# A float32 chain of attention and two expert mixtures: the first mixture by Strassen's block product, token groups outside and experts inside

## The chip, the cores and the metric

The kernel runs on one core of one Trainium2 chip. The metric is the device time of one execution in microseconds (us), taken as the median of several runs. The engines are TensorE (PE, whose weight loads the profile lists as PEld), VectorE (DVE), ScalarE (ACT), GpSimd (POOL) and SyncE (SP, which here only issues DMAs).

## The reference

2304 tokens of 512 features pass through three parts. The first is a causal attention without softmax with a decay per head. Its output `x` goes through a dense mixture of 8 experts, whose weights `P` come from 8 rounds of row and column normalisation. The result goes through a mixture in which each token visits only its best expert.

```python
attn_out = _attn_ref(q, k, v)                      # B, H, S, DH = 4, 8, 576, 64
x = attn_out.transpose(0, 2, 1, 3).reshape(B * S, H * DH)       # 2304 x 512

# first mixture, E = 8, F = 1024: every token through every expert
logits = x @ w_gate
P = np.exp(logits - logits.max())
for _ in range(8):
    P /= P.sum(1, keepdims=True) + 1e-09
    P /= P.sum(0, keepdims=True) + 1e-09
    P *= N / E
for e in range(E):
    out += P[:, e:e + 1] * (np.maximum(x @ w1[e], 0.0) @ w2[e])

# second mixture: every token through its best expert alone
expert_idx = np.argmax(logits2, axis=1)
for e in range(E):
    mask = expert_idx == e
    out[mask] = gate_w[mask, None] * (np.maximum(x[mask] @ w1[e], 0.0) @ w2[e])
```

## The kernel before

All matrix products of the first mixture, and the second product of the second mixture, are made from two float32r halves of each operand: a rounded part (names with H) and the rest (names with L). One product of two tiles costs three matmuls, H by H, H by L and L by H. ACT writes the H part with a copy or a relu, and DVE or POOL subtracts it from the source for the L part.

**First mixture.** The 16 units are half experts (512 of the 1024 hidden features), in the order expert outside, half inside. Each unit runs over 6 blocks of 384 tokens (`BLK`, `NB`). For a block, `hidden` (L1005 to L1012) makes 4 hidden tiles of 128 features, each from 12 matmuls of 384 columns, and `output` (L1014 to L1024) makes 3 output tiles of 128 tokens, each from 12 matmuls of 512 columns. That is 48 and 36 matmuls per block, 96 blocks in all. ACT's `relu_hi` (L535 to L539) writes `HH` from PSUM, DVE's `relu_lo` writes `HL` (L729) and then adds the weighted output tile in PSUM to `acc` (L757). The weights of the next unit are loaded by SP as one MB for each of `w1raw` and `w2raw` (L319, L320) and split by ACT (L553, L556) and by POOL's `split_lo` (L419, L421). Weights are loaded and split once.

**Normalisation of P.** It runs beside blocks 0 to 5 of the first unit. DVE makes row sums and column partials, and POOL adds the partials over the 128 partitions with `partition_all_reduce` (L436), eight times. After every second one POOL also splits a quarter of the next unit's weights:

```python
for it in range(SINK):
    pool.wait_ge(s_cp, it + 1)
    nc.gpsimd.partition_all_reduce(cs[:, :], cp[:, :], P, bass.bass_isa.ReduceOp.add).then_inc(s_cs, 1)
    if it % 2 == 1:
        split_lo(1, 1, it // 2)
```

**Routing.** In the last unit, after block i, the 3 token tiles of block i-1 are complete. PE transposes them and makes the logits, DVE chooses the expert (`choose`) and ranks the tokens (`rank`), and POOL scatters the rows to their sorted places in DRAM.

**Second mixture.** Tokens lie sorted by expert in tiles of 128, 22 tiles in this run. A tile costs PE 32 float32 products (recorded as 64 matmuls, L1082), 4 transposes of the next tile, and 24 matmuls of 512 columns (L1093 to L1095). Expert weights (`Wa`, `Wb`) sit in 2 slots. When a slot's `Wb` has arrived, ACT writes `WbH` (L596), and DVE and POOL each write four of the eight `WbL` blocks (L306), right ahead of the expert's tiles. Waits are counted semaphores on each engine, in an order written out by hand. SP's waits and DMAs are one queue in order.

Of the kernel before, what the change touches and what calls it, by code (L numbers as in the profile page):

```python
# [13 lines left out]

B, H, S, DH = 4, 8, 576, 64
P = 128
D = H * DH
# [8 lines left out]
FH = F // 2  # L45
NF = FH // P
NT = N // P
BLK = 384
NB = N // BLK
TPB = BLK // P  # L50
# [3 lines left out]
SQ = 32  # L54
# [5 lines left out]
PICK = NB - 2  # L60
assert P < PICK * BLK // E


def tables():

# [13 lines left out]
    row = np.concatenate([(E - np.arange(E)).astype(float), thr, N * np.arange(E), np.arange(TAB)])  # L79
    keep = np.concatenate([np.eye(P), (p[:, None] < p[None, :]), np.ones((P, P)),  # L80
                           np.tile(row, (P, 1))], 1)
# [3 lines left out]
def build(nc, qk, kv, wg1, w11, w12, wg2, w21, w22, attn_tab, keep_tab, out):  # L85
    ctx = ExitStack()
    with ctx:
# [7 lines left out]
        at_w = base  # L95
        WSLOT = 4 * 4 * NF * D
        at_x = at_w + 2 * WSLOT
        at_acc = at_x + 2 * 4 * ND * N
        at_raw = at_acc + -(-4 * NT * ROW // 32) * 32
        at_h = at_raw + 2 * 4 * NF * D  # L100
        at_small = at_h + 2 * 4 * NF * BLK

        W1H, W1L, W2H, W2L = [], [], [], []
        a = at_w
        for s in range(2):
            for name, group in (("W1H", W1H), ("W1L", W1L), ("W2H", W2H), ("W2L", W2L)):
                t, a = place(f"{name}{s}", [P, ND, FH], F32R, a)
                group.append(t)
        XH, a = place("XH", [P, ND, N], F32R, at_x)
        XL, a = place("XL", [P, ND, N], F32R, a)  # L110
        acc, _ = place("acc", [P, NT, ROW], F32, at_acc)
        w1raw, a = place("w1raw", [P, ND, FH], F32, at_raw)
        w2raw, a = place("w2raw", [P, NF, D], F32, a)
        HH, a = place("HH", [P, NF, BLK], F32R, at_h)
        HL, a = place("HL", [P, NF, BLK], F32R, a)
# [3 lines left out]
        a = at_acc  # L119
# [3 lines left out]
        for c in range(4):  # L123
            t, a = place(f"QK{c}", [P, 2, G, C], F32, a)
            QK.append(t)
        assert a <= at_raw
        a = at_h + 2 * 4 * ND * P
        for c in range(4, NC):
            t, a = place(f"QK{c}", [P, 2, G, C], F32, a)
            QK.append(t)  # L130
        assert a <= at_small
        a = at_w + WSLOT
        VD, QT, ST, PT, qd = [], [], [], [], []
        for s in range(3):
# [3 lines left out]
            QT.append(t)  # L138
        for s in range(2):
# [4 lines left out]
        for c in range(1, NC):  # L144
            t, a = place(f"qd{c}", [P, G, C], F32, a)
            qd.append(t)
# [1027 lines left out]
```

## Time and profile before

| | us |
|---|---|
| median of 3 runs | 2081.91 |
| lowest, highest | 2078.32, 2091.56 |
| the profiled execution's own time | 2079.77 |
| its span, first to last instruction | 2078.1 |
| PE busy | 2035.7 |
| DVE, ACT, POOL busy | 658.1, 357.7, 310.0 |

The span is what the rows are measured in. The profiled execution takes 1.7 us more than its span. PE's busy time counts overlapping matmuls once, so the duration of one matmul is longer than the distance to the next one, and only the distance between starts tells what a row of matmuls costs. The execution has three stages: attention to 104 us, first mixture to 1736 us, second mixture to the end.

### The profile page before, as it was taken

The numbers are of one execution on the slowest core, as the hardware profiler recorded it, in microseconds if no ns is written. First come the engines' busy times: TensorE is split into PE (matmuls) and PEld (weight loads), VectorE is DVE, ScalarE is ACT, GpSimd is POOL, SyncE is SP. The second block draws the span as 40 slices with busy tenths as digits, with TensorE's granted clock in tenths as the row PEclk, the third lists the DMA queues.
The fourth block names the chain that finished last, engine by engine and source line by source line (L and its number), as shares of the span: only waits on it lengthen the run. The fifth ranks groups of instructions, "written<-read, shape, count | busy, mean of one in ns | idle before, by whom it ended". The sixth has DMA issues, their size and how long they took to land. (4 is left out here: it accounts for less than half of the span.)

```text
span 2078.1 us, 31657 instructions
## 1 busy us (share of the span) xinstructions
PE 2035.7 (98%) x11660; PEld 1836.6 (88%) x11661; DVE 658.1 (32%) x1223; ACT 357.7 (17%) x715; POOL 310.0 (15%) x288
## 2 busy tenths in 40 slices
PE   8999999999999999999999999999999998999997
PEld 7899999888889999988889999998888987998886
DVE  4444332222222222222222222222222346223554
ACT  2311111111111111111111111111111112002121
POOL 5501101010101010101000000001010012112232
PEclk9999999999999999999999999999999999999998
DMA  9701040104000410221031104010400006114452
GB/s 251 207 0 41 0 147 0 40 0 147 3 37 29 118 40 0 70 77 40 0 111 36 40 0 147 0 40 0 147 0 0 16 31 224 40 40 160 147 202 92
DMA packets 63308, 141.44 MB, mean 68 GB/s; under 512 B 6254, under 2 KB 6254, under 8 KB 63280
## 3 DMA queue, kind: packets, MB, share of 16 engines
q1 hardware_dynamic: 58240, 125.56, 19.2%
q0 software_dynamic: 5040, 15.51, 2.2%
q8 instruction: 17, 0.28, 0.1%
q14 instruction: 11, 0.09, 0.0%
HBM read 92.91 MB, written 49.19 MB: 68 GB/s over the span
## 5 line engine op out<-in xcount | busy, mean ns | idle before, releaser
L1009 PE MATMUL bank<-XH,W1H 128*128 (+1 forms) x1536 | 515.7, 336 | 0.0
L1010 PE MATMUL bank<-XL,W1H 128*128 (+1 forms) x1536 | 514.3, 335 | 0.0
L1011 PE MATMUL bank<-XH,W1L 128*128 (+1 forms) x1536 | 513.8, 335 | 0.0
L1022 PE MATMUL bank<-W2H,HL 128*128 128x512 f32 x1152 | 459.1, 398 | 0.0
L1021 PE MATMUL bank<-W2L,HH 128*128 128x512 f32 x1152 | 453.9, 394 | 0.0
L1020 PE MATMUL bank<-W2H,HH 128*128 128x512 f32 x1152 | 453.1, 393 | 0.0
L729 DVE SCALAR_TENSOR_TENSOR HL<-bank,HH 128x384 fp32r<-128x384 f32 x384 | 213.7, 557 | 577.8 <-ACT HH L539 535.4
L539 ACT ACTIVATE HH<-bank 128x384 fp32r<-128x384 f32 x360 | 177.2, 492 | 1266.9 <-PE bank L1011 1266.9
L757 DVE SCALAR_TENSOR_TENSOR acc<-bank,Pw,acc 128x512 f32 x252 | 180.3, 751 | 521.1 <-PE bank L1022 519.5
L1009 PEld LDWEIGHTS bank<-XH,W1H 128*128 128x128 f32 x1536 | 288.3, 188 | 4.2
L1010 PEld LDWEIGHTS bank<-XL,W1H 128*128 128x128 f32 x1536 | 288.4, 188 | 4.0
L1011 PEld LDWEIGHTS bank<-XH,W1L 128*128 128x128 f32 x1536 | 288.4, 188 | 0.0
L419 POOL TENSOR_TENSOR W1L<-w1raw,W1H 128x512 fp32r<-128x512 f32 x64 | 82.5, 1288 | 1260.0 <-ACT W2H L556 1232.1
L1021 PEld LDWEIGHTS bank<-W2L,HH 128*128 128x128 f32 x1152 | 216.3, 188 | 51.4
L1022 PEld LDWEIGHTS bank<-W2H,HL 128*128 128x128 f32 x1152 | 216.2, 188 | 50.2
L1020 PEld LDWEIGHTS bank<-W2H,HH 128*128 128x128 f32 x1152 | 216.2, 188 | 48.1 <-issue 1.0
L1082 PEld LDWEIGHTS bank<-x2T,Wa 128*128 128x128 f32 x1408 | 162.1, 193 | 6.2 <-issue 3.7
L1082 PE MATMUL bank<-x2T,Wa 128*128 128x128 f32 x1408 | 162.8, 277 | 4.2 <-DVE x2T L816 4.2
L421 POOL TENSOR_TENSOR W2L<-w2raw,W2H 128x512 fp32r<-128x512 f32 x64 | 82.1, 1283 | 0.0
L1093 PE MATMUL bank<-WbH,hH 128*128 128x512 f32 x176 | 75.7, 430 | 0.1
L1094 PE MATMUL bank<-WbL,hH 128*128 128x512 f32 x176 | 72.9, 414 | 0.0
L1095 PE MATMUL bank<-WbH,hL 128*128 128x512 f32 x176 | 72.5, 412 | 0.0
(149 smaller groups left out, 1007.6 us busy)
## 6 DMA issues: line engine op xcount, KB each, us to landing
sorted_rows<-blank SPq DMA_DIRECT2D x147, 257.0 KB, 8.7
w1raw<-in_moe_w SPq DMA_DIRECT2D x16, 1024.0 KB, 5.1
w2raw<-in_moe_w SPq DMA_DIRECT2D x16, 1024.0 KB, 8.0
Wa<-in_moe_w SPq DMA_DIRECT2D x8, 2048.0 KB, 7.8
Wb<-in_moe_w SPq DMA_DIRECT2D x8, 2048.0 KB, 10.0
QK<-qk SPq DMA_DIRECT2D x24, 384.0 KB, 9.0
KV<-kv SPq DMA_DIRECT2D x24, 384.0 KB, 10.0
nxt<-sorted_rows POOLq DMA_DIRECT2D x23, 257.0 KB
```

The source lines that it names most:

```text
L419: nc.gpsimd.tensor_tensor(W1L[s][:, j, :], w1raw[:, j, :], W1H[s][:, j, :].bitcast(F32), ALU.subtract).then_inc(s_wlo, 1)
L421: nc.gpsimd.tensor_tensor(W2L[s][:, j, :], w2raw[:, j, :], W2H[s][:, j, :].bitcast(F32), ALU.subtract).then_inc(s_wlo, 1)
L539: nc.scalar.activation(HH[:, j, :], bank[j][:, 0:BLK], ACT.Relu).then_inc(s_hhi, 1)
L729: nc.vector.scalar_tensor_tensor(HL[:, j, :], bank[j][:, 0:BLK], 0.0, HH[:, j, :].bitcast(F32), ALU.max, ALU.subtract).then_inc(s_hlo, 1)
L757: nc.vector.scalar_tensor_tensor(tile, bank[L2B[j]][:, :], weight, tile, ALU.mult, ALU.add).then_inc(s_acc, 1)
L1009: mm(bank[j][:, 0:BLK], W1H[s][:, a, f], xh, start=(a == 0), stop=False)
L1010: mm(bank[j][:, 0:BLK], W1H[s][:, a, f], xl, start=False, stop=False)
L1011: last = mm(bank[j][:, 0:BLK], W1L[s][:, a, f], xh, start=False, stop=(a == ND - 1))
L1020: mm(dst, HH[:, j, tok], W2H[s][:, j, :], start=(j == 0), stop=False)
L1021: mm(dst, HH[:, j, tok], W2L[s][:, j, :], start=False, stop=False)
L1022: last = mm(dst, HL[:, j, tok], W2H[s][:, j, :], start=False, stop=(j == NF - 1))
L1082: last = mm(bank[j // 4][:, (j % 4) * P:(j % 4 + 1) * P], Wa[s][:, a, j * P:(j + 1) * P], x2T[:, a, :], start=(a == 0), stop=(a == ND - 1))
```

## The change

The first mixture is rewritten. The tokens are grouped into 3 groups (`SB`) of 768, the group loop is outside and the expert loop inside. A group consists of two halves of `W` = 384 tokens from different batches. A step handles one group, one expert and a quarter of the hidden features (256). There are 3 x 8 x 4 = 96 steps (`K`). In a step the 256 x 768 hidden block is made by Strassen's scheme (in Winograd's form) over 2 x 2 blocks: 7 block products of 2 x 3 matmuls of 384 columns. The sums of tokens are made once per group (DVE's `x_term`, ACT's `x_hi`, DVE's `x_lo`, POOL's `next_x`). The sums of weights are made in each step by POOL (`w1_sum`), since each weight is now loaded and split three times, once per group. DVE adds the products up with 5 additions per step (`sums_before`, `sums_after`), and the second product of a step is issued inside the next step (`outputs(k - 1, ...)`). It adds only 256 features per pass, so `acc` is updated 6 times per step.

```diff
+            def product(b, s, i, start):
+                for c in range(NK):
+                    blk = WBLK[i][c]
+                    mm(bank[b][:, 0:W], W1H[s][:, blk, :], XH[i][:, c, :], start=start and c == 0, stop=False, ...
+                    mm(bank[b][:, 0:W], W1H[s][:, blk, :], XL[i][:, c, :], ...
+                    last = mm(bank[b][:, 0:W], W1L[s][:, blk, :], XH[i][:, c, :], ...
...
+            def step(k, q, sb=None, route=None, sorted_tile=False):
+                pe.wait_ge(s_w1l, 3 * (k + 1))
+                if not first:
+                    pe.wait_ge(s_hlo, 4 * k - 3)
+                product(BA, s, 0, True).then_inc(s_p1, 1)
+                if not first:
+                    pe.wait_ge(s_c21, k)
+                product(BB, s, 1, True).then_inc(s_p6, 1)
+                if not first:
+                    pe.wait_ge(s_c12, k)
+                product(BC, s, 2, True)
+                pe.wait_ge(s_cs1, k + 1)
+                product(BA, s, 3, False).then_inc(s_p2, 1)
+                pe.wait_ge(s_u2, k + 1)
+                product(BB, s, 4, False).then_inc(s_p7, 1)
+                if not first:
+                    pe.wait_ge(s_hlo, 4 * k)
+                    pe.wait_ge(s_w2l, k)
+                    for t in range(TS):
+                        outputs(k - 1, 1 - s, t, not fixed(k, 1))
+                pe.wait_ge(s_c22, k + 1)
+                product(BC, s, 5, False).then_inc(s_p3, 1)
+                product(BB, s, 6, False).then_inc(s_p4, 1)
```

DVE's order in a step, shortened:

```diff
+            def sums_before(k):
+                dve.wait_ge(s_p6, k + 1)
+                nc.vector.tensor_tensor(c12[:, :], cs1[:, :], bank[BB][:, 0:W], ALU.add).then_inc(s_u2, 1)
+                dve.wait_ge(s_p7, k + 1)
+                nc.vector.tensor_tensor(c22[:, :], cs1[:, :], bank[BB][:, 0:W], ALU.add).then_inc(s_v, 1)
+                nc.vector.tensor_tensor(c22[:, :], c22[:, :], bank[BC][:, 0:W], ALU.add).then_inc(s_c22, 1)
+            def sums_after(k):
+                dve.wait_ge(s_p3, k + 1)
+                nc.vector.tensor_tensor(c12[:, :], c12[:, :], bank[BC][:, 0:W], ALU.add).then_inc(s_c12, 1)
+                dve.wait_ge(s_p4, k + 1)
+                nc.vector.tensor_tensor(c21[:, :], cs1[:, :], bank[BB][:, 0:W], ALU.add).then_inc(s_c21, 1)
+            def hidden_lo(k, i):
+                source = (bank[BA][:, 0:W], c22[:, :], c12[:, :], c21[:, :])[i]
+                dve.wait_ge(s_hhi, 4 * k + i + 1)
+                nc.vector.scalar_tensor_tensor(HL[:, i, :], source, 0.0, HH[:, i, :].bitcast(F32), ...
...
+            # step: sums_before(k); gather 0 to 2 of step k-1; hidden_lo(k, 0); gather 3 to 5;
+            #       hidden_lo(k, 1); sums_after(k); hidden_lo(k, 2); hidden_lo(k, 3)
```

POOL's step prepares the weights of step k+1 and the second weights of step k. `column_sum` is the `partition_all_reduce`. In steps 0, 1 and 2 it is called 2, 3 and 3 times:

```diff
+            def step(k, q, sink=()):
+                sink = list(sink)
+                for i in range(4):
+                    w1_sum(k + 1, i)
+                if sink:
+                    column_sum(sink.pop(0))
+                for i in range(2):
+                    w1_lo(k + 1, (q + 1) % 2, i)
+                if sink:
+                    column_sum(sink.pop(0))
+                w2_lo(k, q % 2)
+                if sink:
+                    column_sum(sink.pop(0))
+                w1_lo(k + 1, (q + 1) % 2, 2)
...
+                    step(step_no(sb, 0, q), q, ((0, 1), (2, 3, 4), (5, 6, 7), ())[q] if sb == 0 else ())
```

SP's loads are now one pair of 512 KB per step, in this order, with five or six of the blank rows' DMAs behind each pair for 28 steps of the first group:

```diff
+            def load_pair(sb, e, q):
+                k = step_no(sb, e, q)
+                sp.wait_ge(s_w1l, 3 * k - 1)
+                load_w1(e, q)
+                sp.wait_ge(s_w2l, k)
+                load_w2(e, q)
...
+                    for i in range(q * FILL // NQ, (q + 1) * FILL // NQ):
+                        sp.dma_start(sorted_rows[...], blank[:, :]).then_inc(s_blank, 16)
```

The gate's logits are no longer made from float32r halves with the gate weights stationary. They are plain float32 products with the tokens stationary and 8 columns moving, 8 calls after each of the last six attention chunks and 24 behind them (72 in all, `gate`), and they land token by token, so DVE's transposes fall away. The attention's output is kept in float32 (`Xf`). Routing works per half group (6 of them). Four are done in the steps q = 1, 2 of the second and third group, two after the last step.

In the second mixture the weights have three slots. DVE makes all eight `WbL` blocks of expert p+2 behind the tiles of expert p, and POOL makes them only for the first expert:

```diff
-                    split_w2_lo(pool, r * 2 + s, s, 0)
-                    send_tiles(r * 2 + s)
...
+                if p + 2 < E:
+                    split_w2_lo(p + 2)
```

## Rows read from the trace of the kernel before

**Rows 1.** The page: busy time and its share of the span, by engine.
```profile
PE 2035.7 (98%) x11660; PEld 1836.6 (88%) x11661; DVE 658.1 (32%) x1223; ACT 357.7 (17%) x715; POOL 310.0 (15%) x288
```

**Rows 2.** Windows: stretch, length, busy us (PE, PEld, DVE, ACT, POOL), clock, DMA share, GB/s.
```profile
0.00:104.20 104.20, 94.23 (x1325) 84.77 (x1327) 47.77 (x104) 34.90 (x78) 58.90 (x64) 0.92 0.86 228
104.20:1620.00 1515.80, 1515.80 (x7611) 1368.12 (x7610) 421.03 (x731) 241.48 (x485) 155.59 (x129) 1.00 0.14 45
1736.00:1763.20 27.20, 21.32 (x139) 18.47 (x139) 19.49 (x52) 5.63 (x12) 10.17 (x10) 0.94 0.47 172
1907.30:2078.10 170.80, 144.26 (x919) 128.83 (x917) 86.85 (x101) 37.45 (x68) 53.39 (x49) 0.91 0.47 164
```

**Rows 3.** Timeline of PE, one block: start, duration (us), engine, line, operation.
```profile
154.38 0.34 PE L1009 MATMUL bank<-XH,W1H 128*128 x1
...
162.73 0.40 PE L1020 MATMUL bank<-W2H,HH 128*128 128x512 f32 x1
...
171.13 0.34 PE L1009 MATMUL bank<-XH,W1H 128*128 x1
```

**Rows 4.** Groups by line: busy us, mean ns of one | idle before.
```profile
L729 DVE SCALAR_TENSOR_TENSOR HL<-bank,HH 128x384 fp32r<-128x384 f32 x384 | 213.7, 557 | 577.8 <-ACT HH L539 535.4 <-ACT HH L587 42.4
L757 DVE SCALAR_TENSOR_TENSOR acc<-bank,Pw,acc 128x512 f32 x252 | 180.3, 751 | 521.1 <-PE bank L1022 519.5
L419 POOL TENSOR_TENSOR W1L<-w1raw,W1H 128x512 fp32r<-128x512 f32 x64 | 82.5, 1288 | 1260.0 <-ACT W2H L556 1232.1 <-issue 27.8
L553 ACT ACTIVATE W1H<-w1raw x56 | 34.9, 624 | 0.0
```

**Rows 5.** Timeline of POOL and DVE between two all-reduces, idle before in brackets.
```profile
140.50 1.28 POOL L419 TENSOR_TENSOR W1L<-w1raw,W1H 128x512 fp32r<-128x512 f32 x1 [6.97 <-issue]
140.61 0.43 DVE L720 TENSOR_REDUCE cp<-Pw 128x8 f32<-128x144 f32 x1
...
148.87 0.42 POOL L436 PARTITION_ALL_REDUCE cs<-cp  x1 [5.83 <-issue]
152.05 0.40 POOL L436 PARTITION_ALL_REDUCE cs<-cp  x1 [2.75 <-DVE cp L720]
```

**Rows 6.** POOL's sequencer at L436, and at L419.
```profile
L436 POOLq MODIFY_POOL_CONFIG  x6: 1/4/4, 143.2 to 181.4; - x6
L419 POOLq MODIFY_POOL_CONFIG  x8: 88/88/88, 133.5 to 190.5; - x8
```

**Rows 7.** DVE's and POOL's weight splits side by side at one change of expert.
```profile
L306 DVE TENSOR_TENSOR WbL<-Wb,WbH x32: 676/685/5884, 1737.2 to 2059.1; 128x512 fp32r<-128x512 f32 x32
...
1909.69 5.88 DVE L306 TENSOR_TENSOR WbL<-Wb,WbH 128x512 fp32r<-128x512 f32 x1
...
1910.06 4.95 POOL L306 TENSOR_TENSOR WbL<-Wb,WbH 128x512 fp32r<-128x512 f32 x4
```

**Rows 8.** Timeline of DVE, results of three tiles in a row.
```profile
1894.27 0.74 DVE L833 TENSOR_SCALAR y<-bank,held 128x512 f32<-128x512 f32 x1
...
1907.34 0.74 DVE L833 TENSOR_SCALAR y<-bank,held 128x512 f32<-128x512 f32 x1
...
1924.66 0.74 DVE L833 TENSOR_SCALAR y<-bank,held 128x512 f32<-128x512 f32 x1
```

**Rows 9.** DMA issues: count, KB each, median us from issue to landing.
```profile
sorted_rows<-blank SPq DMA_DIRECT2D x147, 257.0 KB, 8.7
w1raw<-in_moe_w SPq DMA_DIRECT2D x16, 1024.0 KB, 5.1
w2raw<-in_moe_w SPq DMA_DIRECT2D x16, 1024.0 KB, 8.0
```

**Rows 10.** Timeline: a hand-over from PE to ACT, and the logits of one block.
```profile
1718.93 0.60 PE L1049 MATMUL bank<-ktab,acc 128*128 128x128 f32 x4
1719.13 0.49 ACT L587 ACTIVATE HH<-bank 128x384 fp32r<-128x384 f32 x1 [1.49 <-PE bank L1011]
...
1724.13 2.81 PE L1057 MATMUL bank<-x2c,wg2s 128*32 128x128 f32 x24
```

More of the change, by code:

```diff
@@ L59, with fixed @@
 WARM = 14
-PICK = NB - 2
-assert P < PICK * BLK // E
+PICK = NG - 2
+assert P < PICK * W // E
+NP = 7
+WBLK = ((0, 2), (8, 9), (6, 7), (1, 3), (10, 11), (12, 13), (4, 5))
+def fixed(number, value):
+    return isinstance(number, int) and number == value
 def tables():
@@ L109, in build @@
[L109 to L115, printed above, removed]
+        WB = 4 * D * F // P
+        W1SLOT = 2 * 4 * 2 * NP * P
+        at_sums = base + W1SLOT
+        at_raw = at_sums + 4 * 4 * NK * P
@@ new lines, in _ @@
+            for sb in range(SB):
+                for q in range(NQ):
+                    k = step_no(sb, 0, q)
+                    step(k, q, first=(k == 0), route=2 * sb - 3 + q if sb > 0 and q in (1, 2) else None,
+                         late_x=sb if q == 0 else None)
+                with act.Fori(1, E - 1) as e:
+                    for q in range(NQ):
+                        step(step_no(sb, e, q), q)
+                for q in range(NQ):
+                    step(step_no(sb, E - 1, q), q, last=(q == NQ - 1), sb=sb)
@@ L611, in _ @@
[L611 to L624 removed]
+            relu2_hi(0, (0,))
@@ new lines, in _ @@
+            for t in range(NT - TS, NT - TPB):
+                routing_x(t)
+            routing_exp(NG - 2)
+            for t in range(NT - TPB, NT):
+                routing_x(t)
+            routing_exp(NG - 1)
+            relu2_hi(0, (1,))
+            split_w2_hi(1)
+            act.wait_ge(s_bounds, 1)
+            for p in range(E):
+                start = act.value_load(bounds[0:1, p:p + 1], min_val=1, max_val=MAXT)
+                end = act.value_load(bounds[0:1, p + 1:p + 2], min_val=2, max_val=MAXT)
+                with act.Fori(start, end) as i:
+                    relu2_hi(i, (0, 1))
+                if p + 2 < E:
+                    split_w2_hi(p + 2)
@@ L881, in _ @@
+            dve.wait_ge(s_acc, TS * (K - 1))
+            for t in range(TS - 1):
+                gather(SB - 1, K - 1, E - 1, t, "add")
+            relu2_lo(0, (0,))
+            choose(NG - 2)
+            gather(SB - 1, K - 1, E - 1, TS - 1, "add")
+            rank(NG - 2)
+            choose(NG - 1)
+            rank(NG - 1)
             dve.wait_ge(s_count, 1)
-            link(nc.vector.tensor_copy(count[:, :], bank[7][:, 0:E]))
+            link(nc.vector.tensor_copy(count[:, :], bank[RB][:, COUNT0:COUNT0 + E]))
@@ L1041, in _, with gate @@
-            unit(E - 1, 0)
-            def routing_T(t, dst):
-                pe.wait_ge(s_acc, (2 * E - 1) * NT + t + 2)
+                    chunk(b, c, True)
+            def gate(t):
+                half, at = t % TS // TPB, t % TPB * P
+                for a in range(ND):
+                    last = mm(bank[RB][:, t * E:(t + 1) * E], Xf[t // TS][:, a, half, at:at + P], wgraw[:, a, :],
+                              start=(a == 0), stop=(a == ND - 1), skip_group_check=True)
+                return last
```

1085 lines of the change are left out of this document (623 added, 462 removed).

## The prediction, made before the changed kernel ran

> **What bounds the kernel now.** I read the page first: PE is busy 98% of the span, DVE 32%, POOL 15% [rows 1]. The windows by stage come next. The first mixture lasts from 104.2 to 1736 us, and in its long part PE is busy in every microsecond at a clock of 1.00 [rows 2]. The timeline of PE gives the price of a matmul there. A block runs from 154.38 to 162.73 with 48 matmuls of 384 columns and to 171.13 with 36 of 512, so one costs 8.35/48 = 0.174 us and 8.40/36 = 0.233 us [rows 3]. Blocks of 16.75 us times 96 are 1608 us, and routing beside the last unit makes up the rest. Only fewer matmul slots shorten this stage. Two places matter for what the change may lose. POOL's waits on nothing visible stand beside the all-reduces [rows 5, 6], and DVE and POOL get into each other's way at changes of expert [rows 7, 8]. The last stretch, with seven changes of expert, has a clock of 0.91 and gaps on PE [rows 2].
>
> **1. Matmuls saved.** A step makes 7 x 6 = 42 matmuls of 384 columns and 36 of 512: 42 x 0.174 + 36 x 0.233 = 15.71 us in place of 16.75. Over 96 steps that is -100 us. The operands keep their shapes, so I take the same price.
>
> **2. POOL's all-reduces, steps 0 to 2.** In rows 5, DVE's partial sums are ready at 141.04 and POOL's subtraction pair ends at 143.0, yet the all-reduce stands at 148.87, 5.83 us later, behind no wait. The other way, from an all-reduce to a subtraction, 6.97 us pass. An all-reduce directly after another has no such gap: at 152.05 it waited for DVE alone. POOL's sequencer shows a MODIFY_POOL_CONFIG at exactly these changes, 6 and 8 of them [rows 6]. So each change of kind on POOL costs 5.9 or 7.0 us. Before, PE had six blocks (100 us) of work with weights already split. Now each of the eight all-reduces stands between elementwise work on which the next step's first matmul waits (`s_w1l`).
>
> POOL's subtraction of 512 elements takes 1.29 us [rows 4], thus 0.7, 1.3, 2.5 us for 256, 512, 1024. From the first maximum (gmx) to W1 of step 1: 0.4 + 7.0 + sums 2.7 + (5.9 + 0.4) + (7.0 + 1.9) + (5.9 + 0.4) + (7.0 + 2.5) + 2.5 = 43.6 us. Step 1 has three all-reduces: 2.7 + 6.3 + 8.9 + 6.3 + 9.5 + 6.3 + 9.5 = 49.5, and 2.5 for weights that are only requested when `w2_lo` of step 0 is done: 52. Step 2: 49.5. The gate adds to the start. 12 calls are recorded as 24 matmuls in 2.81 us, 0.117 each [rows 10], so 72 calls are 144. Of these 96 (11.2 us) lie in the last six attention chunks, whose gaps hide some 2, and 48 (5.6 us) follow. Before, the first block began at 104.2 us, after 8.6 us of logits. Now gmx falls at 104.2 - 8.6 + 9.2 + 5.6 + 1 = 111.4, and step 3 may begin at 111.4 + 43.6 + 52 + 49.5 = 256.5. PE's own work up to there is 7.3 + 15.7 + 15.7 = 38.7 us. The term is 256.5 - 104.2 - 38.7 = +114 us. Bounds: below, if POOL paid nothing for the changes, 15 us (gate and start); above, +10 for PE's lower clock after each pause, as in the last stretch [rows 2].
>
> The Trainium skill ("GPSIMD Engine Reference", section Instruction dispatch) says that the first call to a freshly loaded kernel pays about 6 us without a visible instruction. Each single gap here agrees. Read as a cost of the first call only, it would make this term about 25 us; rows 5 show it again at each return, so I go by the rows.
>
> **3. Waits inside a step.** With t = 0 at the first matmul: P1, P6, P5, P2, P7 end at 5.2, the outputs at 13.6, P3 at 14.7, P4 at 15.7. ACT starts 0.20 us after PE has moved on [rows 10]. DVE needs 0.56 us for 384 elements and 0.75 for an update of `acc` [rows 4]: per step 6 x 0.75 + 9 x 0.56 = 9.5 us, under 15.7. POOL needs about 9.7 us, ACT about 6. The tightest link is P6 of the next step, at t = 16.75, which waits for c21 = P4 + 0.20 + 0.56 + 0.1 = 16.55. It holds, by 0.2 us.
>
> Queued ahead of c21 on DVE is `hidden_lo(k, 1)`, due at 14.5. It reads `c22` and `HH`, two SBUF operands, where before L729 read PSUM and one SBUF tile. Rows 7 show what such a read can meet: a DVE subtraction from two SBUF tiles takes 0.68 us in the median, but 5.88 when POOL runs four subtractions in a row (1910.06 to 1915.01), and ends 0.56 us after POOL. POOL's sums of weights run once `w1raw` lands. It is issued behind `w2_lo` (t = 7.1) and `w2raw`; one MB lands in 5.1 us, the second at 8.0 [rows 9]. So I get t = 12.3 and sums to 15.1: `hidden_lo(k, 1)` ends at 15.5, and c21 just holds. With rows of 1 KB the landing may be later; each 0.1 us beyond 12.5 then delays P6 by 0.1, up to 1.0 us at 13.8, after which DVE comes first. In 28 steps five blank DMAs (8.7 us to landing [rows 9]) push the landing to the next step's start, where the sums meet `hidden_lo(k, 2)` and `(k, 3)`; outputs wait for those. Bounds: 0 and 96 x 1.0 = 96 us. I take 15, since my landing is nearer to the near end.
>
> The Trainium skill ("SBUF — State Buffer", section Who interferes with whom) says that a VectorE instruction with two SBUF inputs and a GpSimd instruction that reads SBUF exclude each other. Rows 7 agree for POOL's run of four; its consequence is rival B.
>
> **4. Changes of group, routing, expert load.** At two changes of group DVE makes XL parts (two SBUF operands of 768 elements) between updates of `acc`, while POOL is busy without a gap from t = 4.6 to 15.9 (L parts, next_x, sums). PE's fourth to sixth output tiles wait for these updates: 5 to 12 us each, I take 8, twice. Routing keeps PE's work (five groups of T and logits beside the steps or the last outputs, as before). DVE's choose and rank and the load of 4 MB for the first expert ahead of a `w1raw` may cost 1 to 2 us each: 6 together. Sum +22, bounds 5 and 40.
>
> **5. Second mixture.** Results of tiles come 13.07 us apart, and 17.32 where the expert changes [rows 8]: 4.25 us too long. DVE's four subtractions take 7.7 us there, since POOL's four hold one back [rows 7]. Seven changes cost 30. Now DVE makes all eight alone, at 0.61 us from start to start, 4.9 us, behind the previous tile, and ACT's copies lie an expert ahead. 4.9 us fit between the last result and the first half of the relu, about 4 us later plus slack until T. I leave 0.3 per change: -28; bounds -30 and 0 (should DVE's longer block cost what it cost before). The passage from the last output to the first full tile took 27.2 us with 13 us of tile 0's work in it [rows 2]; half of tile 0's hidden product now goes ahead of the outputs, and two half groups are routed behind: -3, bounds -8 and +8.
>
> **Sum.** Against the profiled execution's own 2079.8 (span 2078.1 + 1.7): 2079.8 - 100 + 114 + 15 + 22 - 28 - 3 = 2100 us. The median of the runs shown, 2081.9, lies 2.1 above the profiled one, less than my terms can resolve. 1% (21 us) is about what a measurement of this kernel can tell from no change. So I forecast 2100, +0.9%: what PE saves, POOL's changes of kind take back.
>
> **Rivals.** A: the all-reduces' cost does not reach PE, because the configuration stays loaded or the gaps lie elsewhere. Then term 2 is 15 to 25 and the time 2000 to 2010, 1990 if term 3 is 0. For it: the 6 us could be paid once. Against: 7 gaps of this size around 8 all-reduces in the trace. Chance 0.13. B: the port. POOL's sums hold DVE's two-SBUF reads in most steps, and PE waits for c21 or for the L parts. It decides from a landing at t = 12.5 on; with 0.5 to 1.0 us per step the time is 2085 + 48 to 96 = 2133 to 2181, slower. For it: rows 7, and a margin of only 0.2 us. Against: POOL's sums leave a gap after the first of four, and stalls shift the phase. Chance 0.27. C: waits in terms 3 and 4 nearly vanish (5 in place of 37): 2068. Chance 0.2. The forecast case, 2080 to 2125, has 0.4. That Strassen's steps do not save their matmuls is excluded by counting.
>
> **How the numbers follow.** Faster by over 1% (below 2061): A and a small part of C, 0.18. Within 1% (2061 to 2103): the rest of C and half of the forecast case, 0.39. Slower: 0.43. The range runs from 2045 (between A and C; A is left out) to 2160 (most of B). The likeliest case has its own 2080 to 2125.
>
> **What would show it.** Right: from 111 to 257 us PE is busy about 39 us, in three pieces with pauses of 30 to 37 us, and MODIFY_POOL_CONFIG appears about 16 times. After that steps are 15.7 to 16.2 us apart, and DVE's mean for `HL` from two SBUF tiles is a little over 0.56 us. Tile results in the second mixture are 13.1 to 13.4 us apart at changes of expert too. Wrong: no pauses before 257 us (A), steps over 16.5 us with long `HL` (B), or result distances of 17 us (term 5).

## The result, and the profile after

The change made the kernel slower. Its median is 2183.43 us (4 runs, 2177.12 to 2195.41) against 2083.18 us of the kernel before (4 runs, 2078.32 to 2091.56) on the same chip: a ratio of 1.048, 95% interval 1.043 to 1.054. In the comparisons of the experiments below the median of the kernel before lay between 2078.6 and 2083.2 us. The profiled execution took 2185.14 us with a span of 2183.5. The forecast was 2100, with a range up to 2160.

From the page of the changed kernel, busy time by engine, and two of the costliest groups (busy us, mean ns of one | idle before, releaser):

```profile
PE 1988.0 (91%) x11180; PEld 1790.1 (82%) x11180; DVE 1154.0 (53%) x1956; ACT 618.6 (28%) x1083; POOL 1075.8 (49%) x907
...
L1206 PE MATMUL bank<-XHa,W1H 128*128 128x384 f32 x960 | 341.9, 356 | 153.9 <-POOL W1L L471 143.9
...
L464 POOL TENSOR_TENSOR Sf<-w1raw 128x256 f32<-128x256 f32 x192 | 149.1, 776 | 443.5 <-DMA w1raw<-in_moe_w 435.9
```

Set beside [rows 1], PE's share fell from 98% to 91%. PE stands 154 us before the first block product of a step, 144 of them for POOL's L parts of the weights (`W1L`, line 471). POOL in turn stands 436 us for `w1raw`. So there are two candidates: POOL's own pace, and the landing of `w1raw`. The windows by stage tell where each holds (columns as in [rows 2]):

```profile
72.00:137.00 65.00, 64.36 (x459) 60.31 (x458) 13.70 (x19) 12.63 (x25) 22.27 (x18) 0.50 0.21 50
137.00:293.00 156.00, 49.04 (x200) 43.91 (x200) 40.53 (x113) 17.38 (x30) 32.14 (x34) 0.63 0.06 20
293.00:832.00 539.00, 487.94 (x2284) 430.51 (x2285) 323.01 (x453) 159.66 (x273) 291.88 (x241) 0.96 0.46 128
832.00:1590.00 758.00, 750.78 (x3815) 678.62 (x3814) 468.94 (x799) 256.61 (x443) 478.71 (x385) 0.99 0.22 72
```

Three stretches lose time, and they do not look alike. From 72 to 137 us PE is busy but for 0.6 us, at a granted clock of 0.50. From 137 to 293 us PE works a third of the time. From 293 to 832 us it lacks a tenth (51 us of gaps), and its clock of 0.96 says that a part of the matmuls ran at the lower level too. After 832 us it is busy 99%.

**The start.** The timeline of PE (start, duration, engine, line, operation) shows the gate of the last attention chunk, the remaining gates and the first block product:

```profile
116.41 3.58 PE L1185 MATMUL bank<-wgraw,Xf 128*128 128x8 f32 x16
...
123.25 13.82 PE L1185 MATMUL bank<-wgraw,Xf 128*128 128x8 f32 x64
136.93 0.67 PE L1206 MATMUL bank<-XHa,W1H 128*128 128x384 f32 x1
```

Sixteen recorded gate matmuls take 3.58 us, 0.22 each and nearly twice the 0.117 us that the prediction took from [rows 10], whose stretch ran at full clock with 128 columns. The 8 columns are not the reason: where the first gates still ran at full clock, in the variant with the sums on TensorE, sixteen of them took 1.95 us. The mixture starts at 136.93 instead of 104.2 [rows 2].

**Steps 0 to 2.** The timeline of POOL in step 0, and its sequencer's row at the all-reduce's line:

```profile
154.51 0.43 POOL L481 PARTITION_ALL_REDUCE cs<-cp  x1 [6.49 <-DVE cp L844]
161.81 1.94 POOL L471 TENSOR_TENSOR W1L<-w1raw,W1H 128x512 fp32r<-128x512 f32 x2 [6.87 <-issue]
```
```profile
L481 POOLq MODIFY_POOL_CONFIG  x16: 1/1/14, 148.2 to 275.2; - x16
```

From the first maximum to step 3 POOL changes its kind 17 times (once behind the maximum and 16 times around the sums' all-reduces), and its sequencer records 34 MODIFY_POOL_CONFIG in all, two for each. Sixteen of the gaps are 5.9 to 7.9 us, near the 5.8 and 7.0 of [rows 5] or somewhat over, and one is 9.1. The gap of 6.49 that is booked on `cp` is of the same size as those behind no wait. DVE's first sum of a step (line 937) dates the steps:

```profile
140.84 0.55 DVE L937 TENSOR_TENSOR c<-cs,bank 128x384 f32<-128x384 f32 x1 [2.72 <-PE bank L1210]
186.21 0.55 DVE L937 TENSOR_TENSOR c<-cs,bank 128x384 f32<-128x384 f32 x1 [26.29 <-PE bank L1210]
240.76 0.55 DVE L937 TENSOR_TENSOR c<-cs,bank 128x384 f32<-128x384 f32 x1 [26.40 <-PE bank L1210]
297.15 0.55 DVE L937 TENSOR_TENSOR c<-cs,bank 128x384 f32<-128x384 f32 x1 [27.57 <-PE bank L1210]
```

The distances are 45.4, 54.5 and 56.4 us; forecast were 43.6, 52 and 49.5. PE starts step 3 at 292.80:

```profile
292.80 0.69 PE L1206 MATMUL bank<-XHa,W1H 128*128 128x384 f32 x1 [37.24 <-POOL W1L L471]
```

Afterwards the same distance is 15.5 us in nearly every step of the second and third group. In steps 3 to 31, which carry the blank's DMAs, it is 15.5 twice and otherwise 16.4 to 21.6: 18.35 in the mean of 29.

**A slow step of the first group.** SP's queue and POOL in the same 20 us:

```profile
541.21 0.41 SPq L358 DMA_DIRECT2D w2raw<-in_moe_w  x1
541.82 3.49 SPq L388 DMA_DIRECT2D sorted_rows<-blank  x5
545.59 0.41 SPq L355 DMA_DIRECT2D w1raw<-in_moe_w  x1
559.53 0.41 SPq L358 DMA_DIRECT2D w2raw<-in_moe_w  x1
```
```profile
538.63 2.41 POOL L476 TENSOR_TENSOR W2L<-w2raw,W2H 128x1024 fp32r<-128x1024 f32 x1 [0.17 <-ACT W2H L624]
540.99 2.39 POOL L471 TENSOR_TENSOR W1L<-Sf,W1H 128x1024 fp32r<-128x1024 f32 x1
551.89 0.74 POOL L464 TENSOR_TENSOR Sf<-w1raw 128x256 f32<-128x256 f32 x1 [8.52 <-DMA w1raw<-in_moe_w]
...
554.80 1.99 POOL L471 TENSOR_TENSOR W1L<-w1raw,W1H 128x512 fp32r<-128x512 f32 x2
556.96 2.40 POOL L476 TENSOR_TENSOR W2L<-w2raw,W2H 128x1024 fp32r<-128x1024 f32 x1 [0.17 <-ACT W2H L624]
```

This is a closed ring, and PE is not in it. The end of `W2L` at 541.04 releases SP, which issues `w2raw`, then five blank DMAs (541.82 to 545.3), and only then `w1raw`, although `w1raw`'s buffer has been free since W1L's second part before 538.6. From there: landing and start of the sums 6.3 us later (551.89), sums 2.9, first L parts 2.2, `W2L` 2.4, and SP again at 559.53. Once round is 559.53 - 541.21 = 18.3 us. That is the mean distance of the steps. Without the blanks the ring would be an estimated 18.3 less 3.8, or 14.5 us, under PE's 15.5.

The 29 steps take 83 us more than at 15.5, and PE's gaps in this window are only 51: the rest is spent in matmuls at the lower clock (0.96 in the window), which fills a part of the wait and is no part of the ring.

**The second mixture.** The timeline of DVE, results of three tiles in a row across a change of expert; and the last output of the first mixture on PE:

```profile
2002.27 0.74 DVE L929 TENSOR_SCALAR y<-bank,held 128x512 f32<-128x512 f32 x1
2015.45 0.74 DVE L929 TENSOR_SCALAR y<-bank,held 128x512 f32<-128x512 f32 x1
2028.63 0.74 DVE L929 TENSOR_SCALAR y<-bank,held 128x512 f32<-128x512 f32 x1
```
```profile
L1231 PE MATMUL bank<-W2H,HL x22: 389/393/400, 1849.7 to 1873.8; 128*128 128x512 f32 x22
```

From the second result on all are 13.18 us apart (the first distance is 15.57); the 17.32 of [rows 8] is gone. First to last result takes 279.2 us (1894.44 to 2173.61), before 305.1.

Where the 105 us of span went, in the prediction's terms:

| term | forecast | measured |
|---|---|---|
| 1 matmuls (15.5 us per step, not 15.71) | -100 | -120 |
| 2 start of the mixture and steps 0 to 2 | +114 | +150 |
| 3 waits inside a step | +15 | +83 |
| 4 groups, routing, expert load | +22 | +25 |
| 5 second mixture; passage | -28; -3 | -26; -7 |
| sum | +20 | +105 |

Term 2: step 3 starts at 292.8; less 104.2 and the 38.7 of PE's own work. Term 3: 29 x (18.35 - 15.5); the last of the 29 crosses the change of group and is 17.8 us even without the blanks ahead of `w1raw`, so some 2 us of it are term 4's. Term 4 is what is left of the span's difference. The distances at the two changes of group (15.5 and 17.7 us over steady steps) and at the expert load (5.4) make 39, and part of that is routing work on PE, which the kernel before had too. Passage: 1894.44 - 1874.2 = 20.2 against 27.1.

### The profile page after: what moved, and what is told of

Read it like the earlier page. It is cut to its first block and busy times, and to the rows that moved or that the text cites. A ratio compares the mean times of both kernels' runs of the same rounds, so it can differ in the third digit from the quotient of the medians.

```text
span 2183.5 us, 32028 instructions
## 1 busy us (share of the span) xinstructions
PE 1988.0 (91%) x11180; PEld 1790.1 (82%) x11180; DVE 1154.0 (53%) x1956; ACT 618.6 (28%) x1083; POOL 1075.8 (49%) x907
## 5 line engine op out<-in xcount | busy, mean ns | idle before, releaser
L972 DVE SCALAR_TENSOR_TENSOR acc<-bank,Pw,acc 128x512 f32<-128x512 f32 x540 | 399.3, 749 | 218.7 <-PE bank L1231 211.2
L1206 PE MATMUL bank<-XHa,W1H 128*128 128x384 f32 x960 | 341.9, 356 | 153.9 <-POOL W1L L471 143.9
L1210 PE MATMUL bank<-XHa,W1L 128*128 128x384 f32 x960 | 333.8, 348 | 0.0
L1208 PE MATMUL bank<-XLa,W1H 128*128 128x384 f32 x960 | 333.5, 347 | 0.0
L1206 PEld LDWEIGHTS bank<-XHa,W1H 128*128 128x128 f32 x960 | 190.6, 199 | 170.9 <-POOL W1L L471 107.6
L476 POOL TENSOR_TENSOR W2L<-w2raw,W2H 128x1024 fp32r<-128x1024 f32 x96 | 230.1, 2396 | 47.7 <-ACT W2H L624 26.2
L471 POOL TENSOR_TENSOR W1L<-Sf,W1H 128x1024 fp32r<-128x1024 f32 x96 | 232.8, 2425 | 14.6 <-issue 14.2
L953 DVE SCALAR_TENSOR_TENSOR HL<-c,HH 128x384 fp32r<-128x384 f32 x288 | 210.7, 744 | 10.7
L1208 PEld LDWEIGHTS bank<-XLa,W1H 128*128 128x128 f32 x960 | 190.8, 199 | 0.0
L1210 PEld LDWEIGHTS bank<-XHa,W1L 128*128 128x128 f32 x960 | 189.5, 197 | 0.0
```

What stands on the lines that cost most here:

```text
L471: nc.gpsimd.tensor_tensor(W1L[s][:, blk, :], raw, W1H[s][:, blk, :].bitcast(F32), ALU.subtract).then_inc(s_w1l, 1)
L476: nc.gpsimd.tensor_tensor(W2L[s][:, :, :], w2raw[:, :, :], W2H[s][:, :, :].bitcast(F32), ALU.subtract).then_inc(s_w2l, 1)
L953: nc.vector.scalar_tensor_tensor(HL[:, i, :], source, 0.0, HH[:, i, :].bitcast(F32), ALU.max, ALU.subtract).then_inc(s_hlo, 1)
L972: ins = nc.vector.scalar_tensor_tensor(tile, psum, weight, tile, ALU.mult, ALU.add)
L1206: mm(bank[b][:, 0:W], W1H[s][:, blk, :], XH[i][:, c, :], start=start and c == 0, stop=False, skip_group_check=True)
L1208: mm(bank[b][:, 0:W], W1H[s][:, blk, :], XL[i][:, c, :], start=False, stop=False, skip_group_check=True)
```

## The experiments

Theory K: the all-reduces between elementwise work cost PE 110 us in steps 0 to 2. Theory L: the blank's DMAs ahead of `w1raw` cost 80 us in steps 3 to 31. Rivals were D (for the first: PE would wait at these places anyway) and P (for the second: the SBUF port between DVE's two-operand reads and POOL's sums, rival B of the prediction).

**The column sums on TensorE.** All eight all-reduces of the sums become one product each with the matrix of ones, issued on PE beside the steps. The one for the maximum stays on POOL. The cut is shortened to the old and the new form of a sum.

```diff
-                nc.gpsimd.partition_all_reduce(cs[:, :], cp[:, :], P, bass.bass_isa.ReduceOp.add).then_inc(s_cs, 1)
...
+                mm(bank[RB][:, CS0:CS0 + E], ones, cp[:, :], start=True, stop=True, ...).then_inc(s_cs, 1)
```

> The eight partition sums of the normalisation are made by PE (ones times the partials, 8 columns, into a free corner of a bank) in place of POOL's all-reduces; only the one for the maximum stays on POOL. Theory K (POOL's changes of kind are the cost): from step 0 to step 3 the distance of 156 us in the changed kernel falls to 55 to 65 us (one change of 7 us, weights of step 1, DVE's chain), so the time is 2183 - 95 = 2088 us, bounds 2075 and 2105. Rival D (the serial chain of row and column sums through DVE is the cost, whoever adds the partials): the distance stays above 120 us and the time above 2145.

Measured: 2093.22 us (10 runs), 1.006 of the kernel before (1.004 to 1.009), 90 us under the changed kernel. The first steps, from the same DVE row as above (line 931 here):

```profile
135.18 0.56 DVE L931 TENSOR_TENSOR c<-cs,bank 128x384 f32<-128x384 f32 x1 [3.10 <-PE bank L1204]
158.82 0.56 DVE L931 TENSOR_TENSOR c<-cs,bank 128x384 f32<-128x384 f32 x1 [0.48 <-PE bank L1204]
180.74 0.55 DVE L931 TENSOR_TENSOR c<-cs,bank 128x384 f32<-128x384 f32 x1 [0.35 <-PE bank L1204]
203.24 0.55 DVE L931 TENSOR_TENSOR c<-cs,bank 128x384 f32<-128x384 f32 x1 [1.19 <-PE bank L1204]
```

68.1 us in place of 156.3, so nearly all of the 90 us lies there. K holds, though the distance is somewhat over the 55 to 65 us expected. 68.1 is still 21.6 over three steady steps, and PE's waits there now are for DVE: 14.1 us for `cp` (12.9 of it in step 0), 4.0 for the hidden sums, 2.9 for `acc`. Steps 3 to 31 stay as slow as before, 18.4 us apart in the mean.

**The all-reduces of a step in one group.** They stay on POOL, but stand behind the step's elementwise work, so that the kind changes 6 times and not 16.

```diff
-                if sink:
-                    column_sum(sink.pop(0))
...
                 w1_lo(k + 1, (q + 1) % 2, 2)
+                for it in sink:
+                    column_sum(it)
```

> POOL keeps its eight all-reduces, but makes those of a step one after the other behind the elementwise work of that step, so that the changes of kind fall from 16 to 6. Theory K: 10 changes of 5.9 to 7.0 us less on POOL, of which the longer chain behind each group gives some back: step 3's start 80 us earlier and step 4's weights some 15 to 20 us late, in all 2183 - 60 = 2123 us, bounds 2105 and 2145. Rival D: the same chain of sums, now later in each step, so 2183 or more.

Measured: 2116.84 us, one run. The step distances are 26.6, 31.5 and 31.9 us, together 90.0: 66 us less for ten changes of kind fewer, 6.6 each. The 68 us between the two profiled executions hold more than that. The mixture begins at 124.50, 12.4 us earlier with the same code ahead of it, which is luck, and steps 3 to 31 take 10.5 us longer. POOL's timeline in step 0:

```profile
148.92 0.43 POOL L481 PARTITION_ALL_REDUCE cs<-cp  x1 [6.06 <-issue]
152.08 0.40 POOL L481 PARTITION_ALL_REDUCE cs<-cp  x1 [2.73 <-DVE cp L840]
159.66 0.74 POOL L464 TENSOR_TENSOR Sf<-w1raw 128x256 f32<-128x256 f32 x1 [7.18 <-issue]
```

The change of kind is the price, not the all-reduce: the second all-reduce waits 2.73 us for DVE alone. A rule of the Trainium skill bears on this ("GPSIMD Engine Reference", section Instruction dispatch): the first call to a freshly loaded kernel pays about 6 us without a visible instruction. The trace shows the size, but at each return to a kind that has run before, and in both directions.

**The blanks behind `w1raw`.**

```diff
-                    load_pair(0, e, q)
+                    k = step_no(0, e, q)
+                    sp.wait_ge(s_w1l, 3 * k - 1)
+                    load_w1(e, q)
                     for i in range(q * FILL // NQ, (q + 1) * FILL // NQ):
                         sp.dma_start(sorted_rows[...], blank[:, :]).then_inc(s_blank, 16)
+                    sp.wait_ge(s_w2l, k)
+                    load_w2(e, q)
```

> In the first group SP issues the five or six blank rows' DMAs of a step behind the first weights' load of that step and ahead of its wait for the second weights' slot; before they stood between the two loads that POOL's next sums wait for. Everything else is the changed kernel. Theory L (the loop through SP, the blank DMAs, the landing of w1raw and POOL's sums and L parts is longer than a step): steps 3 to 31 fall from 18.3 us to 15.5 to 15.8, the time from 2183 to 2103 us, bounds 2095 and 2120. Rival P (the port that DVE's reads from two SBUF tiles share with POOL is the cost, and it is there with or without the late landing): steps stay above 17 us and the time above 2150.

Measured: 2105.98 us (4 runs), 1.011 of the kernel before (1.007 to 1.015), 77 us less than the changed kernel, with the same DMAs and the same bytes. SP's queue, POOL's start of the sums, and the window of the same stretch:

```profile
538.28 0.41 SPq L355 DMA_DIRECT2D w1raw<-in_moe_w  x1
538.90 3.78 SPq L390 DMA_DIRECT2D sorted_rows<-blank  x5
552.65 0.41 SPq L358 DMA_DIRECT2D w2raw<-in_moe_w  x1
```
```profile
544.09 0.74 POOL L468 TENSOR_TENSOR Sf<-w1raw 128x256 f32<-128x256 f32 x1 [4.59 <-DMA w1raw<-in_moe_w]
```
```profile
293.00:832.00 539.00, 532.34 (x2686) 481.57 (x2687) 341.41 (x551) 184.63 (x317) 346.61 (x279) 0.99 0.42 137
```

POOL starts the sums 5.8 us after the issue of `w1raw`, and the steps 4 to 31 are 15.5 us apart but for a few; PE is busy 532 of 539 us (488 before). L holds: it was the place in the queue, not the traffic. The port's part is tried next.

**The read from two SBUF tiles behind the sums.** In DVE's order, `hidden_lo(k, 1)` moves behind `sums_after(k)`, so that nothing with two SBUF operands stands ahead of c21.

```diff
-                hidden_lo(k, 1)
...
                 sums_after(k)
-                for i in range(2, 4):
+                for i in range(1, 4):
```

> In each step DVE makes the L part of the second hidden block (two SBUF inputs) behind the two sums c12 and c21 in place of ahead of them, so that a read held back by POOL no longer holds back c21, on which the next step's second product waits. Rival P: the 28 slow steps lose what the port costs, 1 to 2 us each, so 2130 to 2155 us. Theory L: the weights still come late, 2183 us, within 10.

Measured: 2175.78 us, one run, with a mixture that began 10.5 us earlier (126.48) than in the changed kernel's profile. The rest of the kernel gained nothing: steps 3 to 31 are 18.36 us apart in the mean, as before. The group of these reads from 300 to 830 us, first in the changed kernel, then here:

```profile
L953 DVE SCALAR_TENSOR_TENSOR HL<-c,HH 128x384 fp32r<-128x384 f32 x87 | 86.9, 1024 | 3.5
```
```profile
L953 DVE SCALAR_TENSOR_TENSOR HL<-c,HH 128x384 fp32r<-128x384 f32 x86 | 57.4, 719 | 0.0
```

Something holds these reads: 1024 ns in the mean where the same operation from PSUM takes 556, and 719 with the other order. In the slow step above the long one runs from 541.55 to 543.78, beside POOL's third L part (540.99 to 543.38), and not beside its sums (551.89 to 554.8) as rival B had it. The 30 us less of DVE time bought PE nothing, since the ring above set the step. Rival P falls as the cause. That it is the port that holds the reads fits the trace and was not tested by itself.

**Both edits.** The sums on TensorE and the blanks behind `w1raw`, each as above.

> The changed kernel with both edits that gained by themselves: the eight column sums as TensorE products with a matrix of ones (it gave 90 us back) and the blank's DMAs issued behind w1raw's (it gave 77 us back). If the two costs are of different stretches (the start of the mixture, and steps 3 to 31) as the profile says, they add up: 2183 - 90 - 77 = 2016 us, 2003 to 2035 allowed, below the kernel before. If they are partly one cost (GpSimd as the one late engine in both), the second edit gives less: 2050 to 2085 us. In the profile no step distance in the first group should then be over 16.5 us but the first four.

Measured: 2017.63 us (4 runs), 0.970 of the kernel before (0.967 to 0.973). The two gains add up to within 2 us of the expectation, so the costs are separate. Step distances are 24.7, 21.9, 21.9, 16.6, 15.5, 17.2, and then 15.2 to 15.8 up to the change of group. The wording of the expectation was a little too strict: one distance, 17.2, is over 16.5 behind the first four.

**All gates behind the attention.** What remains is the start, still at 136.61 there. On top of both edits:

```diff
-            early = [t for t in range(NT) if t % TS < TPB or t < TS]
+            early = []
```

> The sums-and-blanks variant with all 72 gates behind the attention instead of some between its last blocks. In the changed kernel the granted clock is 0.50 from about 72 us to 150 us, and the early gates (16 recorded matmuls of 8 columns, 3.58 us for each) run in that stretch. Theory N: the clock falls because of the narrow gate products among the attention's; with them behind it the attention keeps 1.00 and ends earlier, and the gates then run in 17 us (full clock) to 31 us (half): 8 to 25 us under the sums-and-blanks variant, about 2000 us. Theory O: the clock falls in the attention for another reason (TensorE's waits there), then the order changes nothing but the place of the gates: within 5 us of the sums-and-blanks variant, and the clock at 0.50 from about 72 us again.

Measured: 2017.01 us (4 runs), no gain. The gates in PE's timeline:

```profile
98.52 30.68 PE L1183 MATMUL bank<-wgraw,Xf 128*128 128x8 f32 x143 [0.59 <-ACT Xf L606]
```

The clock falls at 79.4 us, 1.9 us after PE had waited 2.47 us and without a gate so far; the attention runs on at 0.50, and the gates behind it too. So the fall here does not need the gates, and moving them gains nothing, as O forecast. (The profiled execution took 2010.56, with a mixture from 129.27.) That does not clear the narrow gates. In the variant with the sums on TensorE the clock was back at 1.00 at 74.8 us, among attention matmuls, and fell again at 78.3, 1.4 us behind its first gates, while PE had no gap:

```profile
74.99 1.95 PE L1179 MATMUL bank<-wgraw,Xf 128*128 128x8 f32 x16
...
81.78 3.58 PE L1179 MATMUL bank<-wgraw,Xf 128*128 128x8 f32 x16
```

**Gates 128 columns wide.** On top of that, each gate's moving operand repeats the 8 weights sixteen times; the further columns are unused.

```diff
-                    last = mm(bank[RB][:, t * E:(t + 1) * E], ..., wgraw[:, a, :],
+                    last = mm(bank[RB][:, t * E:t * E + P], ...,
+                              wgraw[:, a, :].unsqueeze(1).to_broadcast([P, P // E, E]),
```

> As the variant with all gates behind the attention, with each gate product's 8 moving columns repeated to 128 (the same weights read sixteen times, the further 120 columns unused). Theory N (narrow products bring the clock down): the clock stays at 1.00 through the gates, or rises within them; each gate's 16 matmuls then cost what the attention's wide ones cost, and the time is at or under that of the gates-behind variant, down by up to 10 us. Theory O (the width has no part in it): the clock is as in the gates-behind variant, and the wider products at half clock add 72 x 16 x 60 ns, some 50 us or more.

Measured: 2000.47 us (4 runs), 0.961 (0.959 to 0.963). In PE's timeline:

```profile
103.61 18.46 PE L1183 MATMUL bank<-wgraw,Xf 128*128 128x128 f32 x144 [0.59 <-ACT Xf L606]
```

Sixteen times the columns in 60% of the time, since the clock came back to 1.00 at 108.1 us, 4.5 us into them; the narrow ones of the variant before ran 30.7 us at 0.50 to their end. The gain of 16.5 us is more than the 10 that N allowed. O's 50 us had counted 16 matmuls per call where the trace records 2.

The kernel before is no example of either. Its gates of 384 columns stand behind the attention, and its clock had fallen at 70.5 us and was back at 77.4 among attention matmuls alone:

```profile
71.00:77.00 6.00, 6.00 (x52) 5.43 (x54) 1.24 (x3) 0.73 (x3) 3.81 (x4) 0.50 1.04 266
```
```profile
95.58 0.44 PE L1000 MATMUL bank<-XH,WGA 128*128 128x384 f32 x1
```

**Wide gates between the attention chunks.** On top of both edits, with the gates in their old places, 15 of 18 tiles are wide.

```diff
+                    wide = t // TPB != 3
-                    last = mm(bank[RB][:, t * E:(t + 1) * E], ..., wgraw[:, a, :],
+                    last = mm(bank[RB][:, t * E:t * E + (P if wide else E)], ...,
+                              wgraw[:, a, :].unsqueeze(1).to_broadcast([P, P // E, E]) if wide else wgraw[:, a, :],
```

> The sums-and-blanks variant with the gates left where the changed kernel has them (48 calls between the last attention blocks) and 15 of the 18 tiles' gates 128 columns wide by the same repetition (the three tiles whose wide result would cover another's stay at 8 columns). With the wide gates all behind the attention the clock came back to 1.00 within them, while the attention before them still ran at 0.50 from about 77 us. Theory N (narrow products hold the clock down, wide ones let it rise): the clock is back at 1.00 soon after the first wide gates, at 85 to 100 us as in the kernel before; then the attention's last blocks also run at full clock, the mixture starts at 105 to 115 us (121.8 with the wide gates behind, 136.6 in the sums-and-blanks variant) and the time is 1985 to 1997 us. Theory O (the clock comes back by length of uninterrupted work, whatever its width): the clock stays at 0.50 through the attention, each early group of 16 takes 3.6 us or more as before, and the time is 2010 us or above.

Measured: 1993.20 us (4 runs), 0.957 (0.952 to 0.962). Windows, and the three narrow tiles in PE's timeline (one of their 24 matmuls is not recorded):

```profile
76.00:106.00 30.00, 30.00 (x374) 27.81 (x375) 14.13 (x16) 11.36 (x22) 16.10 (x14) 1.00 0.20 52
107.00:109.00 2.00, 2.00 (x11) 2.00 (x11) 0.00 (x0) 0.00 (x0) 0.00 (x0) 0.50 0.00 0
```
```profile
102.80 2.81 PE L1184 MATMUL bank<-wgraw,Xf 128*128 128x8 f32 x23
```

The mixture starts at 109.4. The clock is low for 6.8 us (from 68.8 to 75.7), as in the kernel before, and not for 68. But it was back just before the first wide gate (75.82), so that gate did not raise it. What the wide gates do is seen behind it: through five more chunks of attention and gates the clock stays at 1.00. Then come the three narrow tiles, and at 106.4 it falls once more, for 3.4 us, in a stretch where PE has no gap. The same fall stands behind the same tiles in the next two variants (at 109.0 and 100.0).

**Wide gates alone.** The changed kernel with this edit only.

> The changed kernel with the wider gates alone, the sums on GpSimd and the blank's DMAs as in the change. This prices what the half clock at the start costs by itself. Theory N: the mixture's first matmul comes at 105 to 115 us in place of 136.93, the distances of the first steps (45.4, 54.5, 56.4) stay, since GpSimd sets them, and the time is 2183 less 22 to 32, some 2157 us. Theory O: 2183 or more.

Measured: 2159.50 us (4 runs), 1.037 (1.033 to 1.041): 24 us less than the changed kernel. In its PE timeline 16 recorded gate matmuls take 2.05 us where the narrow ones took 3.58:

```profile
84.91 2.05 PE L1186 MATMUL bank<-wgraw,Xf 128*128 128x128 f32 x16
```

The clock was back at 81.7, 4.0 us into the first wide gates. The mixture starts at 113.3, and the next step distances are 46.2, 56.0 and 54.5 us, much as in the changed kernel. Nothing but the width of 15 of the 18 gates differs, so this prices the half clock at the start: 24 us, by itself.

**The first expert's weights behind `w1raw`.** At step 80 SP issues 4 MB for the second mixture ahead of `w1raw`, and POOL waited 15.4 us for `w1raw` there in the changed kernel. The edit puts them behind it, on top of the variant with both edits and wide gates between the chunks.

```diff
-            load_expert(0)
+            k = step_no(2, E // 2, 0)
+            sp.wait_ge(s_w1l, 3 * k - 1)
+            load_w1(E // 2, 0)
+            load_expert(0)
+            sp.wait_ge(s_w2l, k)
+            load_w2(E // 2, 0)
...
```

> The variant with sums on TensorE, blanks behind w1raw and wide gates between, and the 4 MB of the second mixture's first expert issued behind step 80's w1raw instead of ahead of it. In the changed kernel GpSimd waited 15.4 us there for w1raw, and one step distance is 20.9 us (21.6 and 16.1 in the variant without this edit). Theory Q (the loss is w1raw standing behind the 4 MB): both distances return to 15.5 to 16.3 us, 5 to 6.5 us saved, 1987 us. Theory R (w2raw, now behind the 4 MB, is late instead, since w2l of the same step waits for it): the loss moves one step later and stays at 4 to 7 us, 1993 us.

Measured: 1985.18 us (4 runs), 0.955 of the kernel before (0.949 to 0.960). The intervals of this and the variant without the edit overlap; the steps tell it. The start of the sums on POOL at this place, without the edit and with it:

```profile
1405.08 0.75 POOL L468 TENSOR_TENSOR Sf<-w1raw 128x256 f32<-128x256 f32 x1 [15.81 <-DMA w1raw<-in_moe_w]
```
```profile
1385.04 0.74 POOL L475 TENSOR_TENSOR Sf<-w1raw 128x256 f32<-128x256 f32 x1 [3.03 <-DMA w1raw<-in_moe_w]
```

The two distances of 21.6 and 16.1 us become 15.6 and 15.4. Q holds, with 6.7 us. The profiled execution also began the mixture at 104.0 instead of 109.4, so the 8 us between the medians are not all this edit's. By its median this version is the fastest of all, 4.5% under the kernel before and 9% under the change as it was made.

## Why the prediction was wrong

The forecast was close to no change, and the kernel became 4.8% slower: 85 us over the forecast in the profiled execution. By terms, the waits inside a step (term 3) missed by 68 us and the start with steps 0 to 2 (term 2) by 36. The matmuls (term 1) were 20 us better than forecast, and terms 4 and 5 were near.

Term 3 is the step that failed, and in its pricing, not in what was seen. It said that the five blank DMAs "push the landing to the next step's start", in 28 steps, and then priced only what the late sums would meet on DVE, the port. The question left out was whether the loads of weights, POOL's work on them and the wait of SP for POOL close a ring of their own, and how long once round is. All its parts were in the prediction's own list of durations but one, the time that SP needs to issue five DMAs: 3.5 us from the first to the last, 3.8 with what lies between. 29 steps times 2.85 us is 83 us in place of the 15 taken; the upper bound of 96 had room for it, but for another reason. Removing the blanks from the ring gave 77 us back.

Term 2 was right in its mechanism and near in two of its three steps: 45.4 and 54.5 us for 43.6 and 52. The third was 56.4 for 49.5: its six gaps sum to 45.5 us where three of 5.9 and three of 7.0 were taken, and the longest is 9.1. The steps together were short by 11 us. The larger miss was the start: the prediction put 72 calls, or 144 matmuls, at 0.117 us each. That is what 8 columns cost at full clock too, but the gates ran at half, and the chunks of attention around them did as well. That moved `gmx` from the forecast 111.4 to 137.56, 26 us; wide gates alone gave 24 us back. The prediction's upper bound for this term, +10 "for PE's lower clock after each pause", looked in the pauses behind the start and not before it.

Term 1 erred in the other direction: steady steps are 15.5 us apart and not 15.71, 20 us over the kernel. The timeline of PE in a step of the second group shows which price was off:

```profile
1002.67 0.39 PE L1229 MATMUL bank<-W2H,HH 128*128 128x512 f32 x1
...
1010.87 0.33 PE L1206 MATMUL bank<-XHb,W1H 128*128 128x384 f32 x1
...
1018.17 0.39 PE L1229 MATMUL bank<-W2H,HH 128*128 128x512 f32 x1
```

The 42 product matmuls take 7.30 us, 0.174 each as in [rows 3]; the 36 of 512 columns take 8.20, 0.228 each and not 0.233. Why they are closer together than before was not tested.

Term 4 came out at 25 for 22. The wait of 8 us at each change for XL parts was only partly that; in the variant with both edits PE stands idle for 5.1 us from 655 to 730 us, and the rest of the longer distances there is work on PE, the routing. This was read from the trace and not tested. The expert load ahead of a `w1raw` was put at 1 to 2 us, and is 5.4 in the changed kernel and 6.7 in the last experiment.

Term 5 was right: -26 for -28, with no result 17 us apart any more. The passage is -7 for -3.

Of the rivals, A (the cost of the changes does not reach PE) is refuted by the first two experiments. B reached up to 2181, nearly the right time, by the wrong mechanism: that would have been luck. C was half true: outside the first group the steady steps have no waits. That is where a forecast of a Strassen step should have begun; the two removable costs stood only where other work shares POOL and SP. The prediction's shares by outcome do not quite follow from its rivals' chances: the rest of C and half of the forecast case are 0.35 and not 0.39, which leaves 0.47 and not 0.43 for slower.

## What to carry to other kernels

Where a load, the work on it and the buffer's release form a ring, add up once round, with the issuing engine's time for every DMA that stands ahead of the load, and compare it with the step; a ring longer than the step sets the pace though no engine in it is near full. Issue what is urgent first: here the same DMAs in another order were worth 77 us. Keep all-reduces on GpSimd out of elementwise work or group them; and take a duration for TensorE work only from a stretch whose granted clock is the one that you expect.

## What was not expected of the hardware

PE was busy 64.4 of the 65 us from 72 to 137 us, and the granted clock stayed at 0.50, the lower of its two levels (1.2 of 2.4 GHz). The matmuls there have 64 to 96 columns (attention) and 8 (gates). With the gates at 128 columns in the same places and nothing else changed, the clock was back at 1.00 at 81.7 us and stayed there to 109 us, behind the three tiles that kept 8 columns. The Trainium skill ("TensorE: Matmul & The Clock Gate", section "Part 1: The HAM clock gate (the "warmup" mystery)") says that activity releases the throttle. The wide gates agree; with the narrow ones PE worked for 65 us at the lower level.

Set side by side, the twelve traces show two kinds of occasion on which the clock fell near the end of the attention. In eight of them it fell in a wait of PE of 1.9 to 2.9 us or within 2.1 us behind one, and in a ninth (wide gates behind the attention) behind two waits of 0.7 and 0.8 us. In six traces (the two experiments of a single run at 72 to 73 us, the sums on TensorE at 78.3, and the last three variants at 100 to 109 us) it fell behind gates of 8 columns while PE had no gap. Between chunks with gates of 128 columns it never fell. The attention's own matmuls are an open point: in the kernel before and in two variants the clock rose among them before any gate, but with all gates behind the attention it stayed at 0.50 through 19 and 26 us of them, with waits of at most 1.1 us. In profiled executions with narrow gates between the chunks the mixture started anywhere from 124.5 to 136.9 us with the same code ahead of it, so a single execution says little about the start.

GpSimd stood idle for 5.9 to 7.9 us at sixteen of the changed kernel's 17 changes between an all-reduce and elementwise work (9.1 at the other), in both directions, however often both had run; ten changes fewer were worth 66 us.
